# Token routing between attention and a mixture of experts: scatters ahead of gathers, weight splits moved, ranks in bf16

## The chip, the cores and the metric

The kernel runs on one core of a Trainium2 chip. The metric is the device time of one execution in microseconds (us); lower is better. The core has five engines that run their own instruction streams and meet at semaphores: TensorE (PE), VectorE (DVE), ScalarE (ACT), GpSimd (POOL) and SyncE (SP), which here only issues transfers.

## What is computed

The reference, cut to what matters:

```python
# attention, q, k, v: (4, 8, 576, 64)
scores = scale * q @ k.T
scores = where(scores >= max(scores) - tau, scores, -1e9)
x = (softmax(scores) @ v)                    # -> (2304, 512)
# mixture of experts: w1 (8, 512, 1024), w2 (8, 1024, 512)
logits = x @ w_gate                          # (2304, 8)
expert_idx = argmax(logits, axis=1)
gate_w = softmax(logits)[expert_idx]
for e in range(8):
    xe = x[expert_idx == e]
    out[expert_idx == e] = gate_w * (maximum(xe @ w1[e], 0) @ w2[e])
# second network: w_in (512, 2048), w_out (2048, 512)
h = out @ w_in
result = (h - tanh(h)) @ w_out
```

Each token goes to exactly one expert, and which one is known only after attention.

## The kernel before

**Stages.** Attention runs over 16 pairs of heads (`PAIRS`), each in 9 units of score rows. Then comes the routing, then the experts in 25 tiles of 128 token rows (`ITEMS` = 18 + 7: the rows of an expert start at a multiple of 128), then the second network in 9 groups of 256 rows. All matrix products that matter are made in three passes of a high and a low part of each operand; so every weight chunk (128 x 2048, `CHUNK`, four for each expert) has to be split into both parts in the `ring`: a copy that rounds (high, L557) and a subtraction (low, L559), both on GpSimd for the experts.

**Attention's end.** VectorE's `scale_rows` writes the attention rows to `x_sb` and, for each head, its part of the gate logits to `lg_parts`; each counts up `x_ready`. SP's `keep_batch` copies `x_sb` to the DRAM tensor `x_tokens`, the last batch after the last `x_ready`. ScalarE issues the zero fill of `x_sorted` (`clear_rows`, L1391) near the end of attention.

**Routing, a chain on VectorE (L1176 to L1263).** The helper `step` makes each instruction wait for the one before. In order: the late logits (L1176, the last six token tiles over all eight heads), maximum, shift, `onehot` (one-hot expert for each token), `run_in` (a running count along the 18 tiles in each partition), `run_ex` (L1205). TensorE then makes three fp32 products (L942 to L944): the rank of each token among those of its expert, and the count of each expert. From the counts VectorE works out how many tiles each expert takes (`ntile`, `tile_end`), the first slot of each (`base`), the slot of each token (`slot_of`, `pos`, `pos_u` at L1226, which releases `pos_ready`). After that it finds which tokens stand in the first three tiles (`PICKED` = 3): `item_of`, `lane_of`, `in_item`, `row_at` (L1229 to L1238), and `lanes` (L1241, two instructions of nine token tiles each). TensorE multiplies `lanes` with `row_at` (L950, 18 bf16 products), VectorE turns the result into row numbers, `item_rows` (L1252 to L1255). Beside them stand the map from tile to expert (`tile_end_i` L1245, `item_e_i` L1249) and the first output row of each tile (`row0_i`, L1263).

**GpSimd's queue in this stretch (L708 to L741).** When attention is over it issues the loads of chunks 4 and 5 into `raw_mid`, splits both (`split_mid`), waits for `map_ready` and `rows_ready`, gathers the rows of the first three tiles straight from `x_tokens` (L721, indirect DMA), and only then scatters all 18 token tiles to their slots in `x_sorted` (L730, indirect DMA). After that it splits the other chunks as SP loads them (L734 on); SP starts these loads when all scatters have landed, since they land in `x_sb` (`raw_late`).

**The experts.** TensorE turns the rows of a tile (`turn_rows`, L963), ScalarE and VectorE make the high and low part (`high_xT` L1522, `low_xT` with the helper at L1267), TensorE multiplies (`up`, L974), ScalarE applies the maximum (`relu`, L1527), TensorE turns again (`turn_hidden`, L984), both parts are made again (`high_hT` L1532, `low_hT`), TensorE multiplies (`down`, L996). The first three tiles are written out, the others loop. `up` of expert e waits for the first half of its chunks in `w_ready`, `down` for all. Tiles from the fourth on are loaded from `x_sorted` by ScalarE (`load_rows`, L1518).

## Time and profile before

| | us |
|---|---|
| median of 3 runs | 1127.73 (1126.7 to 1131.57) |
| the profiled execution | 1136.3 |
| its span, first to last instruction | 1134.6 |
| TensorE busy | 1048.8 (92%) |
| VectorE busy | 680.0 (60%) |
| ScalarE busy | 454.2 (40%) |
| GpSimd busy | 779.9 (69%) |

The profile is of one execution, and all times below are in us from the start of its span. Busy time of TensorE is modelled at the ends of its instructions. A page by 40 slices shows TensorE at 90% or more in nearly all slices but those from 340 to 400 us, the routing stretch. A line of a timeline is: start, duration (us), engine, source line, operation, output and input tiles, shapes, number of instructions, and in brackets the idle time of the engine before it with what ended it.

### The profile page before, as it was taken

How to read it: one execution, taken by the hardware profiler on the slowest of the kernel's cores; microseconds unless marked ns; L12 is line 12 of the kernel's file. 1: busy time of each engine (PE TensorE's matmuls, PEld its weight loads, DVE VectorE, ACT ScalarE, POOL GpSimd, SP SyncE). 2: the span in 40 equal slices, each digit the busy share in tenths (PEclk: the TensorE clock that was granted, in tenths of full speed). 3: DMA queues.
4: the chain of work that ended last, by engine and by line, in shares of the span. 5: the costliest groups of instructions: out<-in, count | busy, mean ns of one | idle time of the engine just before them, and what ended most of it. 6: DMA issues, size and time to landing. Idle time of an engine off the chain costs nothing.

```text
span 1134.6 us, 19577 instructions
## 1 busy us (share of the span) xinstructions
PE 1048.8 (92%) x6428; PEld 874.4 (77%) x6429; DVE 680.0 (60%) x1240; ACT 454.2 (40%) x865; POOL 779.9 (69%) x731
## 2 busy tenths in 40 slices
PE   3999999999983389999999999989999999999997
PEld 2677767777762368888888888879989999999995
DVE  2777777777765413232224223877877877778774
ACT  2777777777751011221221223333333333333332
POOL 6788888766622763888699731667777776777774
PEclk9999999999997689999999999999999999999999
DMA  4444464533473362545466451000010010100000
GB/s 95 119 120 125 105 178 99 135 96 84 126 255 116 112 251 95 188 145 191 139 235 191 139 176 57 10 19 20 19 37 19 19 37 0 37 19 19 18 10 28
DMA packets 98295, 110.13 MB, mean 97 GB/s; under 512 B 62464, under 2 KB 62464, under 8 KB 97728
## 3 DMA queue, kind: packets, MB, share of 16 engines
q1 hardware_dynamic: 84320, 77.64, 23.9%
q10 hardware_dynamic: 10256, 19.46, 4.9%
q0 software_dynamic: 3664, 12.34, 2.9%
q8 instruction: 28, 0.46, 0.2%
q14 instruction: 27, 0.22, 0.1%
HBM read 67.42 MB, written 27.32 MB: 84 GB/s over the span
## 4 chain that ended last, share of the span: by engine, by line
PE 76%; DVE 7%; POOL 7%; issue 6%; ACT 2%; DMA 1%; SPq 0%; POOLq 0%; ACTq 0%; DVEq 0%
PE ps L1018 17%; PE ps L1035 15%; PE ps L996 12%; PE ps L974 11%; PE ps L845 5%; PE ps L810 5%; PE ps L824 5%; PE ps L984 2%; POOL k_low L603 2%; POOL q_dup L590 1%; PE ps L831 1%; PE ps L857 1%; POOL thresh L610 1%; PE ps L963 1%; DVE lanes L1241 1%
## 5 line engine op out<-in xcount | busy, mean ns | idle before, releaser
L1018 PEld LDWEIGHTS ps<-x2T,ring 128*128 128x128 f32 x1728 | 217.2, 193 | 12.4 <-DVE x2T L1267 7.6
L1018 PE MATMUL ps<-x2T,ring 128*128 128x256 f32 x1728 | 220.1, 284 | 5.6 <-DVE x2T L1267 5.6
L1035 PE MATMUL ps<-ring,gT 128*128 128x512 f32 x864 | 210.3, 392 | 1.6 <-DVE gT L1267 1.6
L1035 PEld LDWEIGHTS ps<-ring,gT 128*128 128x128 f32 x864 | 157.6, 188 | 32.6 <-issue 1.8
L996 PE MATMUL ps<-ring,hT 128*128 x600 | 146.1, 399 | 4.3 <-DVE hT L1267 3.8
L756 POOL TENSOR_SCALAR x_sb<-h_sq 128x512 f32<-128x512 f32 x72 | 144.3, 2005 | 6.1
L974 PE MATMUL ps<-ring,xT 128*128 x600 | 144.6, 397 | 3.4 <-DVE xT L1267 3.4
L753 POOL TENSOR_SCALAR poly<-h_sq 128x512 f32<-128x512 f32 x72 | 48.4, 672 | 133.7 <-ACT h_sq L1560 123.6
L559 POOL TENSOR_TENSOR ring<-x_sb,ring 128x2048 fp32r<-128x2048 f32 x30 | 138.5, 4616 | 2.5
L1102 DVE SCALAR_TENSOR_TENSOR probs<-ps,thresh,probs 128x576 f32<-128x576 f32 x144 | 115.6, 813 | 38.6 <-ACT probs L1420 25.7
L996 PEld LDWEIGHTS ps<-ring,hT 128*128 128x128 f32 x600 | 112.6, 191 | 28.2 <-issue 5.5
L810 PE MATMUL ps<-k_hl,q_dup 128*128 128x288 f32 (+1 forms) x640 | 118.7, 316 | 15.7 <-DMA k_hl<-k_low 12.1
L974 PEld LDWEIGHTS ps<-ring,xT 128*128 128x128 f32 x600 | 112.3, 191 | 26.2 <-issue 4.0
L1094 DVE TENSOR_REDUCE neg_max<-ps 128x1 f32<-128x576 f32 x144 | 106.7, 750 | 30.6 <-PE ps L810 30.2
L1420 ACT ACTIVATE probs<-ps,neg_max 128x576 f32<-128x576 f32 x144 | 104.8, 740 | 17.0 <-DVE neg_max L1094 16.1
L810 PEld LDWEIGHTS ps<-k_hl,q_dup 128*128 128x128 f32 (+1 forms) x640 | 93.2, 192 | 17.1 <-issue 15.9
L755 POOL TENSOR_TENSOR poly<-poly,h_sq 128x512 f32<-128x512 f32 x72 | 98.2, 1364 | 6.0
L1568 ACT ACTIVATE gT<-poly 128x512 fp32r<-128x512 f32 x72 | 45.6, 634 | 140.1 <-PE ps L1035 94.7
L1560 ACT ACTIVATE h_sq<-ps 128x512 f32<-128x512 f32 x72 | 43.0, 597 | 138.1 <-PE ps L1018 138.1
L557 POOL TENSOR_SCALAR ring<-x_sb 128x2048 fp32r<-128x2048 f32 x30 | 57.2, 1907 | 58.1 <-SPq L525 30.0
L824 PE MATMUL ps<-ident,probs 128*128 128x128 f32 x576 | 90.6, 280 | 6.4 <-ACT pT_b L1446 4.1
L1532 ACT ACTIVATE hT<-ps 128x512 fp32r<-128x512 f32 x50 | 27.3, 596 | 164.3 <-DVE y_sb L1291 134.9
(162 smaller groups left out, 1492.6 us busy)
## 6 DMA issues: line engine op xcount, KB each, us to landing
x_sb<-in_moe_w_dram SPq DMA_DIRECT2D x26, 1024.0 KB, 5.9
q_dup<-q_dup SPq DMA_DIRECT2D x32, 288.0 KB, 3.7
x_sorted<-y_sb ACTq DMA_DIRECT2D x1, 6425.0 KB, 21.5
y_ranked<-y_sb ACTq DMA_DIRECT2D x25, 256.5 KB, 3.6
xs<-x_sorted ACTq DMA_DIRECT2D x22, 257.0 KB, 2.8
k_hl<-k_low SPq DMA_DIRECT2D x32, 160.0 KB, 2.4
xs<-y_ranked SPq DMA_DIRECT2D x8, 513.0 KB, 3.7
q_in<-in_q_dram SPq DMA_DIRECT2D x32, 128.0 KB, 2.7
```

Source lines behind the costliest of these rows:

```text
L559: pool.tensor_tensor(ring[:, low:low + CHUNK], raw, ring[:, high:high + CHUNK].bitcast(F32), ALU.subtract).then_inc(w_ready, 1)
L755: pool.tensor_tensor(poly[:, b, :], poly[:, b, :], h_sq[:, b, :], ALU.mult).then_inc(poly_ready, 1)
L756: pool.tensor_scalar(is_large[:, b, :], h_sq[:, b, :], T_SQ, None, ALU.is_ge).then_inc(large_ready, 1)
L810: mm = pe.matmul(scores_of(n)[0:rows, c, :], q_dup[:, s, a, f, cols], k_hl[:, s, a, k0 + c * CH:k0 + (c + 1) * CH], start=(f == 0), stop=( ...
L824: mm = pe.transpose(turn_bank[:, j * P:(j + 1) * P], probs_of(n)[:, k0 + j * P:k0 + (j + 1) * P], ident[:, :])
L974: mm = pe.matmul(psS[:, 0, n, :], xT[:, px, c * P:(c + 1) * P], ring[:, bass.ds(lo + (pw * SLOT + c * F + n * 512), 512)], start=(c == 0 a ...
L996: mm = pe.matmul(psO[:, 0, :], hT[:, px, c * P:(c + 1) * P], ring[:, bass.ds(lo + (pw * SLOT + DC * F + c * DM), DM)], start=(c == 0 and p ...
L1018: mm = pe.matmul(hid(b)[:, fc * GW:(fc + 1) * GW], ring[:, at:at + P], x2T[:, px, c, :], start=(c == 0 and px + pw == 0), stop=(c == DC - ...
L1035: mm = pe.matmul(out_bank(j), gT[:, b % 2, px, cols], ring[:, at:at + DM], start=(b == 0 and fc == 0 and px + pw == 0), stop=(b == NB - 1 ...
L1094: dve.tensor_reduce(neg_max[:, n % 4:n % 4 + 1], scores_of(n), AX.XY, ALU.max, negate=True).then_inc(nmax_ready, 1)
L1102: dve.scalar_tensor_tensor(out=by_halves(probs_of(n)), in0=scores_of(n), scalar=thresh[:, b:b + 1], in1=by_halves(probs_of(n)), op0=ALU.is ...
L1420: act.activation(by_halves(probs_of(n)), scores_of(n), ACT.Exp, bias=neg_max[:, n % 4:n % 4 + 1]).then_inc(exp_ready, 1)
```

## The change

Eight edits. Scatters: the first four of the 18 are issued when `pos_ready` is up, then come the three gathers, then the other 14. Chunks 4 and 5 are loaded by SP during the last pair of attention (with the tensors in the ring laid out anew to make room), their high halves are made by ScalarE (`high_mid`), and GpSimd makes the low halves behind the scatters. The late logits are reduced over six heads before the last `scale_rows`, and the last two heads are added afterwards. `run_ex` falls away: `before` becomes a matrix of 0 and -1, so that the inclusive count serves. The count product is the first of three, all in bf16, with a release of its own. Tile counts are rounded by adding and subtracting a large constant instead of by integers. Small tensors of the last steps lie in PSUM (`route_bank`). The picked rows are summed in one column by 36 products instead of 18, and VectorE copies them out in one step. TensorE waits for `row0_ready` before the first tile, ScalarE no longer waits for `w_ready`.

```diff
@@ sync
                     keep_batch(p // HP - 1)
+            last = PAIRS - 1
+            sp.wait_ge(scores_ready, UNITS * last)
+            sp.wait_ge(raw_trans, 3 * PAIRS)
+            sp.wait_ge(q_split, 2 * PAIRS)
+            sp.wait_ge(k_split, 2 * PAIRS)
+            for a in range(2):
+                sp.wait_ge(k_spread[last % 2][a], 16 * (last // 2 + 1))
+            for j in range(CHUNKS, EARLY):
+                sp.dma_start(chunk_like(raw_mid[:, j % 2, :], ...), ...).then_inc(mid_landed[j % 2], 16)
             keep_batch(B - 1)
@@ gpsimd
             def split_mid(j):
-                pool.wait_ge(mid_landed[j % 2], 16 * ((j - CHUNKS) // 2 + 1))
-                split(*divmod(j, CHUNKS), raw_mid[:, j % 2, :])
+                pool.wait_ge(w_high, j + 1)
+                pool.tensor_tensor(ring[:, low:low + CHUNK], raw_mid[:, j % 2, :],
+                                   ring[:, high:high + CHUNK].bitcast(F32), ALU.subtract).then_inc(w_ready, 1)
...
-            for j in range(CHUNKS, EARLY):
-                if j == CHUNKS:
-                    pool.wait_ge(x_ready, 2 * PAIRS)
-                pool.dma_start(chunk_like(raw_mid[:, j % 2, :], ...), ...).then_inc(mid_landed[j % 2], 16)
-            for j in range(CHUNKS, EARLY):
-                split_mid(j)
+            pool.wait_ge(s_zero_filled, 16)
+            pool.wait_ge(token_numbers, 5)
+            pool.wait_ge(x_ready, 2 * PAIRS)
+            pool.wait_ge(pos_ready, 1)
+            for t in range(BEFORE_PICKED):
+                sort_tile(t)
             pool.wait_ge(x_kept, 32 * B)
-            pool.wait_ge(map_ready, 2)
             pool.wait_ge(rows_ready, 1)
             for t in range(PICKED):
                 pool.indirect_dma_start(...)
...
-            for t in range(TILES):
-                pool.indirect_dma_start(out=x_sorted[:, :], ...).then_inc(x_scattered, 16)
+            for t in range(BEFORE_PICKED, TILES):
+                sort_tile(t)
+            for j in range(CHUNKS, EARLY):
+                split_mid(j)
@@ tensor
-            pe.matmul(psO[:, 1, 0:E * TILES], before[:, :], onehot[:, :, :], start=True, stop=False)
-            pe.matmul(psO[:, 1, 0:E * TILES], ones[:, :], run_ex[:, :, :], start=False, stop=True)
-            pe.matmul(psT[:, 0, 0:E], ones[:, :], run_in[:, :, TILES - 1], start=True, stop=True
+            pe.matmul(psT[:, 0, 0:E], ones_b[:, :], run_in[:, :, TILES - 1], start=True, stop=True
+                      ).then_inc(ranks_ready, 1)
+            pe.matmul(psO[:, 1, 0:E * TILES], not_before[:, :], onehot[:, :, :], start=True, stop=False)
+            pe.matmul(psO[:, 1, 0:E * TILES], ones_b[:, :], run_in[:, :, :], start=False, stop=True
                       ).then_inc(ranks_ready, 1)
             for t in range(TILES):
                 pe.wait_ge(lanes_ready, t // HT + 1)
-                mm = pe.matmul(psS[:, 1, 0, 0:2 * PICKED], lanes[:, t, :], row_at[:, t, :, :]...)
+                for x in range(2):
+                    mm = pe.matmul(psS[:, 1, 0, 0:PICKED], lanes[:, t, :], row_at[:, t, x, :], ...)
...
             pe.wait_ge(map_ready, 2)
+            pe.wait_ge(row0_ready, 1)
             turn_rows(0, first_rows[0])
@@ vector
+            late_heads = route_bank[:, 320:...]
+            half_item, item_of, lane_of = (route_bank[:, x * 32:x * 32 + TILES] for x in range(3))
+            in_item = route_bank[:, 128:...]
...
                     gate_logits(0, FULL - JT).then_inc(logits_ready, 1)
+                    dve.wait_ge(x_ready, 2 * (PAIRS - 1))
+                    dve.tensor_reduce(logits[:, FULL - JT:, :], lg_parts[:, FULL - JT:, 0:H - 2, :]..., AX.X, ALU.add)
                 if past:
                     scale_rows(p - 1, 1)
...
-            gate_logits(FULL - JT, TILES).then_inc(logits_ready, 1)
+            step(dve.tensor_tensor(late_heads, lg_parts[:, FULL - JT:, H - 2, :], lg_parts[:, FULL - JT:, H - 1, :], ALU.add))
+            step(dve.tensor_tensor(logits[:, FULL - JT:, :], logits[:, FULL - JT:, :], late_heads, ALU.add))
...
-            dve.tensor_tensor(run_ex[:, :, :], run_in[:, :, :], onehot[:, :, :], ALU.subtract).then_inc(runs_ready, 1)
+            dve.sem_inc(runs_ready, 1)
...
-            step(dve.tensor_scalar(count_i[:, :], psT[:, 0, 0:E], float(P - 1), float(P), ALU.add, ALU.max))
-            step(dve.tensor_scalar(ntile_i[:, :], count_i[:, :], P.bit_length() - 1, None, ALU.arith_shift_right))
-            step(dve.tensor_copy(ntile[:, :], ntile_i[:, :]))
+            step(dve.tensor_scalar(counts[:, 0, :], psT[:, 0, 0:E], 1.0, (P - 1) / 2, ALU.max, ALU.add))
+            step(dve.tensor_scalar(counts[:, 1, :], counts[:, 0, :], 1 / P, WHOLE, ALU.mult, ALU.add))
+            step(dve.tensor_scalar(ntile[:, :], counts[:, 1, :], WHOLE, None, ALU.subtract))
...
-            step(dve.tensor_scalar(item_of_i[:, :], pos_u[:, :].bitcast(I32), P.bit_length() - 1, None, ALU.arith_shift_right))
-            step(dve.tensor_copy(item_of[:, :], item_of_i[:, :]))
+            step(dve.tensor_scalar(half_item, pos[:, :], (P - 1) / 2, 1 / P, ALU.subtract, ALU.mult))
+            step(dve.tensor_scalar(item_of, half_item, WHOLE, WHOLE, ALU.add, ALU.subtract))
...
             dve.tensor_copy(tile_end_i[:, :], tile_end[:, :]).then_inc(map_ready, 1)
+            dve.wait_ge(rows_psum, 1)
+            dve.tensor_copy(item_rows[:, :], psS[:, 1, 0, 0:PICKED]).then_inc(rows_ready, 1)
+            # then item_ge, item_e, item_e_i, wasted, item_ge, lost, row0, row0_i
@@ scalar
+            act.wait_ge(x_ready, 2 * PAIRS)
+            act.wait_ge(w_high, CHUNKS)
+            high_mid(CHUNKS)
             act.wait_ge(lshift_ready, 1)
             act.activation(lexp[:, :, :], logits[:, :, :], ACT.Exp).then_inc(lexp_ready, 1)
+            for j in range(CHUNKS + 1, EARLY):
+                high_mid(j)
...
             act.wait_ge(map_ready, 2)
-            act.wait_ge(w_ready, EARLY)
             act.wait_ge(row0_ready, 1)
```

`high_mid(j)` waits for `mid_landed` and copies `raw_mid[:, j % 2, :]` to the high part of the ring, then counts up `w_high`; `sort_tile(t)` is the scatter of one token tile, as it was.

## Rows read from the trace of the kernel before

**Rows 1.** The page's first line.
```profile
span 1134.6 us, 19577 instructions
```

**Rows 2.** Windows by stage: stretch, us, busy of each engine, TensorE clock, DMA share, GB/s.
```profile
357.00:365.00 8.00, 1.52 (x6) 1.46 (x6) 6.29 (x22) 0.00 (x0) 1.89 (x1) 0.50 0.85 302
...
460.00:712.00 252.00, 252.00 (x1262) 211.76 (x1260) 76.36 (x126) 60.96 (x106) 176.68 (x59) 1.00 0.48 161
```

**Rows 3.** Timeline of VectorE, 340 to 430 us.
```profile
352.80 0.42 DVE L1117 TENSOR_TENSOR x_sb<-ps,rec 128x256 f32<-128x256 f32 x1 [8.53 <-PE ps L857]
...
353.75 0.84 DVE L1133 TENSOR_REDUCE logits<-lg_parts 128x48 f32<-128x384 f32 x1
...
357.18 0.31 DVE L1205 TENSOR_TENSOR run_ex<-run_in,onehot 128x144 f32<-128x144 f32 x1
...
359.27 0.17 DVE L1214 TENSOR_SCALAR count_i<-ps 128x8 int32<-128x8 f32 x1 [1.05 <-PE ps L944]
...
361.81 0.18 DVE L1226 CAST pos_u<-pos 128x18 uint32<-128x18 f32 x1
...
362.65 0.22 DVE L1234 TENSOR_TENSOR in_item<-item_of,item_no 128x54 f32<-128x54 f32 x1
...
363.16 1.86 DVE L1238 TENSOR_SCALAR row_at<-in_item,partition_no 128x54 bf16<-128x54 f32 x1
365.06 8.66 DVE L1241 TENSOR_TENSOR lanes<-lane_of,lane_no 128x1152 bf16<-128x1152 f32 x2
373.64 4.46 DVE L1245 CAST tile_end_i<-tile_end 128x8 int32<-128x8 f32 x1
...
379.23 0.17 DVE L1255 CAST item_rows<-picked_rows 128x3 uint32<-128x3 f32 x1
...
380.27 0.21 DVE L1263 CAST row_i<-row 128x25 int32<-128x25 f32 x1
...
396.29 0.69 DVE L1267 TENSOR_TENSOR xT<-ps,xT 128x512 fp32r<-128x512 f32 x1 [9.97 <-issue]
```

**Rows 4.** Timeline of GpSimd, 320 to 480 us.
```profile
363.08 1.89 POOL L557 TENSOR_SCALAR ring<-raw_mid 128x2048 fp32r<-128x2048 f32 x1 [7.30 <-DMA raw_mid<-in_moe_w_dram]
365.05 4.49 POOL L559 TENSOR_TENSOR ring<-raw_mid,ring 128x2048 fp32r<-128x2048 f32 x1
369.52 3.00 POOL L557 TENSOR_SCALAR ring<-raw_mid 128x2048 fp32r<-128x2048 f32 x1
372.60 5.47 POOL L559 TENSOR_TENSOR ring<-raw_mid,ring 128x2048 fp32r<-128x2048 f32 x1
380.26 1.10 POOL L721 DMA_INDIRECT xs<-x_tokens,item_rows  x1 [2.19 <-DVE item_rows L1255]
...
406.01 0.97 POOL L730 DMA_INDIRECT x_sorted<-x_sb,pos_u  x1 [0.30 <-issue]
```

**Rows 5.** Timeline of TensorE, 345 to 430 us.
```profile
373.78 0.40 PE L950 MATMUL ps<-row_at,lanes 128*128 128x6 bf16 x9 [2.56 <-DVE lanes L1241]
383.79 1.08 PE L963 MATMUL ps<-ident,xs 128*128 128x128 f32 x4 [9.61 <-DMA xs<-x_tokens,item_rows]
...
407.20 1.45 PE L996 MATMUL ps<-ring,hT 128*128 x4 [3.78 <-DVE hT L1267]
409.03 7.67 PE L996 MATMUL ps<-ring,hT 128*128 x20 [0.38 <-issue]
...
423.26 5.71 PE L996 MATMUL ps<-ring,hT 128*128 x24
```

**Rows 6.** Timeline of ScalarE, second half of the first hidden tile.
```profile
405.56 0.60 ACT L1532 ACTIVATE hT<-ps 128x512 fp32r<-128x512 f32 x1 [5.06 <-remote]
```

**Rows 7.** Timeline of GpSimd, first split of expert 2's chunks.
```profile
447.67 1.91 POOL L557 TENSOR_SCALAR ring<-x_sb 128x2048 fp32r<-128x2048 f32 x1 [19.24 <-SPq L525]
```

**Rows 8.** DMA issues, 310 to 345 us and the page: line, engine, count, size, us to landing.
```profile
x_sorted<-y_sb ACTq DMA_DIRECT2D x1, 6425.0 KB, 21.5
x_tokens<-x_sb SPq DMA_DIRECT2D x4, 1024.0 KB, 4.9
```

More of the change, by code:

```diff
@@ L54, in attention_moe_mlp @@
     PICKED = 3
+    BEFORE_PICKED = 4
     LAG = 3
@@ L128, in attention_moe_mlp @@
         zeros = y_sb
-        (before, ones, logits, lmax, lexp, lsum, rev, pick, pick_max, onehot, keep, item_no, item_ge, item_e,
-         run_in, run_ex, count_i, ntile_i, ntile, tile_end, base, slot_of, pos, lane_no, tile_no, partition_no,
-         picked_rows, item_of_i, item_of) = at_once([
+        (before, not_before, ones_b, logits, lmax, lexp, lsum, rev, pick, pick_max, onehot, keep, run_in, slot_of,
+         item_no, item_ge, item_e, counts, ntile, tile_end, base, ones, pos, lane_no, tile_row, partition_no) = at_once([
             ("before", [P, P], F32),
-            ("ones", [P, P], F32),
+            ("not_before", [P, P], BF16),
+            ("ones_b", [P, P], BF16),
             ("logits", [P, TILES, E], F32),
@@ L146, in attention_moe_mlp @@
             ("item_e", [P, ITEMS], F32),
-            ("run_in", [P, E, TILES], F32),
-            ("run_ex", [P, E, TILES], F32),
-            ("count_i", [P, E], I32),
-            ("ntile_i", [P, E], I32),
+            ("counts", [P, 2, E], F32),
             ("ntile", [P, E], F32),
@@ L949, in _ @@
                 pe.wait_ge(lanes_ready, t // HT + 1)
-                mm = pe.matmul(psS[:, 1, 0, 0:2 * PICKED], lanes[:, t, :],
-                               row_at[:, t, :, :].rearrange("p x i -> p (x i)"),
-                               start=(t == 0), stop=(t == TILES - 1))
+                for x in range(2):
+                    mm = pe.matmul(psS[:, 1, 0, 0:PICKED], lanes[:, t, :], row_at[:, t, x, :],
+                                   start=(t == 0 and x == 0), stop=(t == TILES - 1 and x == 1))
             mm.then_inc(rows_psum, 1)
```

133 lines of the change are left out of this document (70 added, 63 removed).

## Prediction

> **What bounds the kernel now.** I first read the page of the profile for the shares, then the windows by stage, then the chain of waits in order of time, and last the timelines of the single engines around the place where TensorE is idle. The span is 1134.6 us [rows 1]. In the expert stage TensorE has no idle time at all: busy 252.00 of 252 us at full clock [rows 2]. So nothing that the change does to ScalarE, VectorE or GpSimd there can show, unless it makes TensorE wait. The place that counts is the routing between attention and the first expert tile. From 357 to 365 us TensorE is busy for 1.52 of 8 us at a granted clock of 0.50, its 1.2 GHz level [rows 2]. The chain runs through VectorE from 353.75 (the late logits) to 379.40 (`item_rows`, 379.23 + 0.17), then through the first gather of GpSimd at 380.26, and TensorE turns its rows at 383.79 [rows 3 to 5]. What follows is bound by TensorE, so a shift of that 383.79 should reach the end of the kernel whole.
>
> In that chain the eye falls on three VectorE steps. A copy of 54 elements per partition takes 1.86 us, two of 1152 take 8.66 together, one of 8 elements takes 4.46 [rows 3], while their neighbour L1234 of 54 elements takes 0.22. GpSimd is splitting weights from 363.08 on, and the ends fit to 0.1 us: L1238 ends at 365.02, GpSimd's first split instruction at 364.97; the last split ends at 378.07, `tile_end_i` at 378.10 [rows 3, 4]. The second `lanes` step releases TensorE at 373.78 [rows 5], 1.26 after the third split instruction ended (372.52), so a `lanes` step alone costs about 1.2. The engines take turns for whole instructions. The Trainium skill (SBUF — State Buffer, "Who interferes with whom") says the same of a VectorE step with two SBUF inputs, or of a copy or cast between SBUF tensors; by that rule, the trace agrees.
>
> **The change, part by part.** All times are on the axis of the profiled execution.
>
> (a) Late logits. The reduction of 384 elements (0.84 at 353.75) becomes two additions of 48 elements on the path, priced by L1234 (54 elements, 0.22, and 0.02 to the next): 0.48 in place of 0.87, so -0.39. The six other heads are reduced before the last `scale_rows`, in an idle stretch of 8.53 us before 352.80 [rows 3]: at most 0.84, hidden ten times over.
>
> (b) `run_ex` goes: -0.32 (357.18 to 357.50). VectorE then idles 1.05 before L1214 for the three fp32 products [rows 3]. Now one bf16 product of 8 columns must land within the three softmax steps (some 0.8 us). Nine bf16 products of such a size take 0.40 [rows 5]; I take the idle time as gone. At worst it stays: 0 to -1.05.
>
> (c) Five steps of 8 elements in place of seven. From 359.27 to 360.69, the start of L1222, seven take 1.42, so two less give -0.41. The magic-number rounding costs the same per step. Positions are now ready at 361.99 (361.81 + 0.18) [rows 3]; (a) to (c) give -2.17: 359.82.
>
> (d) GpSimd's queue. Today it is: two chunk loads, two splits, three gathers, 18 scatters. After the change: four scatters, three gathers, 14 scatters, two half splits. The indirect DMAs start every 1.29 us ((406.01 - 380.26) / 20), and the first came 0.86 after its release (379.40 to 380.26) [rows 3, 4]. So: first scatter 359.82 + 0.86 = 360.68; four take 5.15: 365.83; the first gather starts then; its rows reach TensorE 3.53 later (380.26 to 383.79): **369.4 in place of 383.8**. The gather now lies behind four scatters in its queue: between nothing and one period, 1.29. I take nothing, since a scatter is issued only every 1.29 us. The gathers' other condition, the kept copy, is issued at x_ready and takes 4.9 [rows 8]; done near 359.5.
>
> (e) Whether the picked rows are known by then. From 359.82: three steps of 18 elements (0.21 each, by L1226), three of 54 (0.25): 361.2. Two `lanes` steps of 1.2: 363.6. Products for the second half are 18 now, not 9: 0.80 and 0.1 of hand-over: 364.5. One copy out of PSUM in place of three steps: 364.8 [rows 3, 5]. That is 1.0 us ahead of the gather, so the four scatters and not VectorE set the gather's start; the longer list of products costs 0.4, which this 1.0 covers.
>
> (f) TensorE now also waits for `row0_ready`, with eight map steps after `item_rows`. Today's steps of that kind take 0.2 to 0.36; eight come to 2.3: 367.1, against 369.4. Hidden by 2.3 us; nothing is queued behind this wait on TensorE but the first item.
>
> (g) Chunk loads on SP during the last pair. They come after the loads of v; in the queue behind them is only the last kept copy, due at 353.7. The zero fill of 6.4 MB needs 21.5 us at that time [rows 8]; 2 MB more lengthens it by about a third, 7 us, so to some 344, still 16 before the first scatter. No cost. The added constant on GpSimd at the start, two short steps, is not on the chain I read; I take 0, at most 0.3.
>
> (h) ScalarE makes the high halves. One of 2048 elements per partition is at most four times 0.60 (512 elements, [rows 6]) = 2.4, from 353.75 to 356.2; then `lexp`, 0.3, used near 356.9. Hidden by 0.4; the bound of the miss is 0.5. GpSimd's two low halves, 4.5 each [rows 4], now start after the scatters, at 365.83 + 17 x 1.29 = 387.7, and end near 397. Expert 1 uses them only after the tiles of expert 0: today GpSimd waits until 447.67 for SP's release of expert 0's first half (SPq L525) [rows 7]. 50 us of margin.
>
> **Sum.** 369.4 - 383.8 = -14.4 us (a shift of the start, not the sum of the single steps). With the bounds of (b), (d) and (h): -14.4 to -11.6; below, -15.2, if the 0.86 before the first indirect DMA is mostly the wake-up of a queue whose other conditions now come first. The profiled execution took 1136.3 us, so 1121.9. It is 8.6 above the median of the runs shown, 1127.73; I keep that distance: **1113.3**.
>
> **The rivals.**
>
> *Late releases shrink* (faster still). In [rows 6] ScalarE's copy of the second half of the first hidden tile starts at 405.56 after 5.06 us that no engine's record explains. TensorE then idles 3.78 before 407.20, and the 24 products run to 416.70, 9.5 in place of 5.71 with a warm clock [rows 5]. That is 7.6 us, beside the scatters, which end at 407 [rows 4]. Now 14 and not 18 scatters lie beside the first items. If the stall goes whole: 1105.7. Against: TensorE's first items and the remaining scatters start together as before; and the profiled run is 8.6 over the median, so the stall may not be in the timed runs.
>
> *Descriptors take turns with VectorE* (less gain). Splits and VectorE's steps within SBUF exclude each other in [rows 3, 4]; the indirect DMAs may do so too. Five map steps have only SBUF operands (`item_ge` twice, `item_e_i`, `row0`, `row0_i`), each exposed to a descriptor step of 0.97: row0 is ready at 367.1 + 4.9 = 372.0, TensorE starts 2.6 later: 1115.9. Against it: L1263 took 0.21 at 380.27, right beside the gather that ran from 380.26 to 381.36 [rows 3, 4]. The Trainium skill (SBUF — State Buffer, "SBUF: two separate sides") states this rule for software DMAs beside copies within SBUF; it speaks against putting scatters beside the map steps, and that one row does not bear it out.
>
> *Late releases reach the start* (much less gain). The 5.06 of [rows 6] could strike the event of the last picking product, since four scatters now run beside it, and once more that of the first turned tile. Rows would be known at 369.9, TensorE would start 3.53 later, 373.5, and lose 5.06 again: 9.2 of the 14.4 are gone: 1122.5. Against: today TensorE's first tile, up to 396.29, meets no such wait beside the first 12 scatters [rows 3].
>
> *Every VectorE step waits for a descriptor step* (slower). If steps with one SBUF operand are caught too, ten steps to `item_rows` take 12.9: 372.7; the gathers then stand behind four scatters and rows land at 377; eight map steps end at 383.0. So the 14 us are gone; and seven VectorE steps of items 0 and 1, up to 0.97 each beside 14 scatters, add 6.8: 1127.7 - 0.7 + 6.8 = 1133.8. It decides from 0.97 per step in about 20 of the 25 steps. Against: the step at 396.29, one operand in PSUM, took its ordinary 0.69 in the middle of the scatters [rows 3, 4].
>
> **How the numbers follow.** Forecast 57% (1112.5 to 1116.1), stall gone 20% (1105.7), map steps held 12% (1115.9), late start 8% (1122.5), slower 3% (1133.8). The range takes in the first three, with 1 and 3 us for the distance between profiled and timed: 1105 to 1119. About 0.5% (5.6 us) is what a measurement can tell from no change; below 1122.1 lie the first three and a quarter of the fourth: 91%; within 7%; slower by more 2%.
>
> **What would show it.** Right: `pos_u` ends near 359.8, the two `lanes` steps take 1.2 each, no VectorE step of 8 elements takes over 0.3, first scatter at 360.7, TensorE's first L963 at 369.4, the expert stage without idle time. Wrong: `item_rows` later than the fourth scatter's end; `row0_i` after the gather's landing; any new idle time of TensorE at expert 1's first tile; a stall at the hidden tile of another length than before.

## The result, and where its time lies

The kernel before takes 1129.78 us (median of five runs, 1126.7 to 1131.57), the changed kernel 1119.27 us (median of five, 1118.12 to 1121.1): the ratio is 0.9912, with an interval of 0.9891 to 0.9933. That is 10.5 us less. The forecast was 14.4 us less, 1113.3 us; the measured time lies 0.3 us above the upper end of its range. Of the 6.0 us between 1113.3 and 1119.27, 2.05 are the base (the forecast started from 1127.73, the median of three runs, and five give 1129.78); the other 3.9 are gain that did not come.

The profiled execution of the changed kernel took 1119.28 us. The first line of its page:

```profile
span 1117.5 us, 19613 instructions
```

Against [rows 1] the span is 17.1 us shorter, more than the 10.5 of the timed medians. Two places make it up. TensorE's first tile is turned at 373.55 and not at 383.79 [rows 5], which is 10.24 earlier. From there to the end of the first item's second matrix (the product with `hT`) it takes 25.2 us and not 32.9. That second difference of 7.7 is the stall of [rows 6], which the profiled execution of before has and that of after does not. After it both need nearly the same, 717.9 and 718.8 us. So 10.24 is the change's own part, and it agrees with the timed 10.5. The profiled execution of before (1136.3) lay 6.5 us above the median of its five timed runs, and the stall is of that size; that the timed runs mostly went without it is inferred from this and not shown.

VectorE's timeline of the changed kernel, from the last attention output to the end of the map (start, us, line, operation, operands; in brackets the idle time before it and what ended it):

```profile
354.58 0.22 DVE L1209 TENSOR_TENSOR ps<-lg_parts 128x48 f32<-128x48 f32 x1
...
356.70 0.78 DVE L1222 TENSOR_TENSOR onehot<-pick,pick_max 128x144 bf16<-128x144 f32 x1
357.52 0.46 DVE L1226 TENSOR_TENSOR_SCAN run_in<-keep,onehot 128x144 bf16<-128x144 f32 x1
358.12 0.30 DVE L1231 TENSOR_REDUCE lsum<-lexp 128x18 f32<-128x144 f32 x1
...
358.96 0.17 DVE L1237 TENSOR_SCALAR counts<-ps 128x8 f32<-128x8 f32 x1
...
361.09 0.18 DVE L1248 CAST pos_u<-pos 128x18 uint32<-128x18 f32 x1
...
362.34 0.28 DVE L1259 TENSOR_SCALAR row_at<-ps,partition_no 128x54 bf16<-128x54 f32 x1
362.65 2.62 DVE L1262 TENSOR_TENSOR lanes<-ps,lane_no 128x1152 bf16<-128x1152 f32 x2
...
365.19 0.16 DVE L1265 CAST tile_end_i<-tile_end 128x8 int32<-128x8 f32 x1
366.01 0.16 DVE L1268 CAST item_rows<-ps 128x3 uint32<-128x3 f32 x1 [0.66 <-PE ps L965]
...
368.07 0.20 DVE L1282 CAST row_i<-row 128x25 int32<-128x25 f32 x1
```

The long steps of [rows 3] are gone: `row_at` takes 0.28 in place of 1.86, the two `lanes` steps 2.62 together in place of 8.66, and `tile_end_i` 0.16 in place of 4.46. The item rows are known at 366.17, 4.90 after the positions (361.27); before it was 17.4 (361.99 to 379.40).

GpSimd and TensorE of the same execution:

```profile
364.50 1.23 POOL L726 DMA_INDIRECT x_sorted<-x_sb,pos_u  x1 [20.72 <-issue]
366.03 0.98 POOL L726 DMA_INDIRECT x_sorted<-x_sb,pos_u  x1 [0.30 <-issue]
...
369.86 0.99 POOL L739 DMA_INDIRECT xs<-x_tokens,item_rows  x1 [0.30 <-issue]
...
373.55 1.09 PE L977 MATMUL ps<-ident,xs 128*128 128x128 f32 x4 [7.58 <-DMA xs<-x_tokens,item_rows]
...
393.01 5.72 PE L1010 MATMUL ps<-ring,hT 128*128 x24
```

The first scatter starts 3.23 us after the positions are ready. That is the one large surprise, and the chain of waits shows it as time in which nothing is seen to run:

```profile
361.09 0.19 DVE pos_u L1248
...
361.30 0.04 POOLq L733
361.35 3.15 issue
364.50 1.23 POOL x_sorted L726
```

GpSimd's sequencer passed its wait for the positions (L733) at 361.30, and 3.15 us later the first scatter began. From there on all goes by the forecast: the fourth scatter ends, the gather follows, its rows land, TensorE turns them.

### The profile page after: what moved, and what is told of

Read it like the earlier page. It is cut to its first block, busy times and chain, and to the rows that moved or that the text cites. A ratio compares the mean times of both kernels' runs of the same rounds, so it can differ in the third digit from the quotient of the medians.

```text
span 1117.5 us, 19613 instructions
## 1 busy us (share of the span) xinstructions
PE 1046.8 (94%) x6443; PEld 873.4 (78%) x6444; DVE 666.2 (60%) x1238; ACT 457.5 (41%) x867; POOL 771.9 (69%) x729
## 3 DMA queue, kind: packets, MB, share of 16 engines
q0 software_dynamic: 3120, 10.24, 2.5%
## 4 chain that ended last, share of the span: by engine, by line
PE 77%; POOL 9%; DVE 6%; issue 5%; ACT 2%; DMA 1%; SPq 0%; POOLq 0%; ACTq 0%; DVEq 0%
PE ps L1032 17%; PE ps L1049 16%; PE ps L988 13%; PE ps L1010 12%; PE ps L858 5%; PE ps L837 4%; PE ps L823 4%; POOL k_low L618 2%; PE ps L998 2%; POOL q_dup L605 2%; POOL thresh L625 1%; PE ps L844 1%; PE ps L870 1%; PE ps L977 1%; POOL k_hl L616 1%
## 5 line engine op out<-in xcount | busy, mean ns | idle before, releaser
L1010 PE MATMUL ps<-ring,hT 128*128 x600 | 143.0, 394 | 0.0
L1355 DVE SCALAR_TENSOR_TENSOR poly<-poly,h_sq 128x512 f32<-128x512 f32 x72 | 50.6, 703 | 71.1 <-POOL poly L768 71.1
## 6 DMA issues: line engine op xcount, KB each, us to landing
x_sorted<-y_sb ACTq DMA_DIRECT2D x1, 6425.0 KB, 26.5
```

Source lines behind the costliest of these rows:

```text
L1010: mm = pe.matmul(psO[:, 0, :], hT[:, px, c * P:(c + 1) * P], ring[:, bass.ds(lo + (pw * SLOT + DC * F + c * DM), DM)], start=(c == 0 and p ...
```

## The experiments

Three things were open: what the 3.15 us are, which part of the change brings the gain, and whether the stall of [rows 6] belongs to one order of the GpSimd queue. For the first there were three theories. **Cold queue**: the first software DMA after a long idle time of GpSimd takes three microseconds to start. **VectorE**: the item steps of VectorE, which run without a gap behind `pos_u`, keep GpSimd from making the descriptors. **Code fetch**: the code of GpSimd behind the wait isn't loaded yet when the wait ends.

### The kernel before, once more

No edit; it shows how the stall varies.

> The kernel before once more, unchanged, to see whether its stall at the first hidden tile (TensorE idle 3.8 us before down(0), its 24 products 9.5 us instead of 5.7) stands in every execution. Theory A, the stall belongs to the profiled execution only by chance: it is absent or of another length here, and the span is up to 7 us shorter than 1134.6. Theory B, it belongs to the kernel: the ScalarE copy of the second hidden half again starts some 5 us late, and the span is within 2 us of 1134.6.

One run took 1139.55 us; the kernel before, timed eleven times in this series, had a median of 1137.1 us (1133.85 to 1139.0), some 7 us above the 1129.78 of the first. The stall is there again. ScalarE's copies out of the first hidden tile, and TensorE behind them:

```profile
401.88 0.60 ACT L1532 ACTIVATE hT<-ps 128x512 fp32r<-128x512 f32 x1 [4.38 <-remote]
408.91 0.60 ACT L1532 ACTIVATE hT<-ps 128x512 fp32r<-128x512 f32 x1 [6.43 <-remote]
...
410.55 8.28 PE L996 MATMUL ps<-ring,hT 128*128 x24 [4.24 <-DVE hT L1267]
```

The copy of the second half waits for 6.43 us. The one semaphore that ScalarE waits for there, `hT_psum`, is counted up by TensorE's turning products (L984), and the last of these ended at 396.52, 12.4 us before the copy starts; no engine's record explains the time between. TensorE idles 4.24 and then runs its 24 products at 8.28 in place of 5.71. Positions came 8.27 after the last attention output, as in the first profile.

### One indirect DMA ahead of the wait for the positions

```diff
             pool.wait_ge(x_ready, 2 * PAIRS)
+            pool.wait_ge(warm, 1)
+            pool.indirect_dma_start(
+                out=warm_dst[:, :], out_offset=None, in_=w_gate[:, :],
+                in_offset=bass.IndirectOffsetOnAxis(ap=warm_rows[:, 0:1], axis=0)).then_inc(warmed, 16)
             pool.wait_ge(pos_ready, 1)
...
             pool.wait_ge(x_kept, 32 * B)
+            pool.wait_ge(warmed, 16)
             pool.wait_ge(rows_ready, 1)
```

> The changed kernel with one small gather (8 numbers per partition, its result is not used) issued by GpSimd as soon as attention is over, before it waits for the positions. In the changed kernel the first scatter starts 3.2 us after the positions are ready, not 0.86. Theory 1, a first indirect DMA costs some 2.4 us once, or GpSimd has to wake from a long idle stretch: the small gather pays it, the first scatter starts about 0.8 us after the positions, TensorE's first tile comes 2.4 us earlier, and the time falls by 2.4 us against the changed kernel. Theory 2, VectorE's steps beside it hold GpSimd up: still 3.2 us, and no change of the time.

Measured: 1118.81 us, ratio 0.9848 (0.9827 to 0.987) to the 1137.1 of its series.

```profile
358.88 1.24 POOL L739 DMA_INDIRECT warm_dst<-in_moe_w_gate_dram,warm_rows  x1 [14.18 <-issue]
362.69 1.01 POOL L731 DMA_INDIRECT x_sorted<-x_sb,pos_u  x1 [2.56 <-DVE pos_u L1258]
```

The first scatter now starts 0.29 after the positions (362.40). The 3.2 us have moved to the dummy gather: its wait for the attention output ended at 355.71, and it started 3.17 later. Both "cold queue" and "code fetch" say this, so the run excludes only "VectorE" as the sole cause. TensorE begins 16.82 after the last attention output, in the changed kernel 18.99. The changed kernel was not timed in this series, so what this is worth in time is not known.

One more row of this kernel matters below:

```profile
368.12 0.16 DVE L1278 CAST item_rows<-ps 128x3 uint32<-128x3 f32 x1 [1.64 <-PE ps L975]
```

The last picking product ended at 367.10, and VectorE's copy of its result starts 1.02 later. In the changed kernel that is 0.04 (365.97 and 366.01). So a late release struck on the way to TensorE's start here, and the gather had to wait 1.57 for the rows.

### The gathers ahead of all scatters

```diff
-    BEFORE_PICKED = 4
+    BEFORE_PICKED = 0
```

> The changed kernel with no scatter ahead of the three gathers (BEFORE_PICKED 0). Picked rows are known at 366.1 in the profile of the changed kernel, the first gather starts at 369.86. Theory 1 (a start-up of about 3.2 us for whatever indirect DMA comes first after idling): the gather starts at about 369.3, the gain is 0.5 us at most. Theory 2 (VectorE's lanes steps delay the first one): it starts 0.9 to 1.3 us after the rows, near 367.2, and TensorE begins 2.7 us earlier; the last scatter ends at most 4 us later than before, which no one waits for.

```profile
367.44 1.23 POOL L739 DMA_INDIRECT xs<-x_tokens,item_rows  x1 [23.35 <-DVE item_rows L1268]
```

GpSimd had been idle for 23.35 us, longer than in the changed kernel (20.72), and yet its first indirect DMA started 0.91 after the rows were known (366.53). "Cold queue" falls with this row: the same first use of the queue after the same idle costs 0.9. What differs is that GpSimd had passed the wait for the positions 5 us before and stood at the next one. The DMA view between 361.5 and 364 us has one packet in it, and it is an instruction packet:

```profile
GB/s 0 0 0 0 0 0 0 0 0 0 0 0 0 0 0 0 0 0 0 0 131 0 0 0 0 0 0 0 0 0 0 0 0 0 0 0 0 0 0 0
...
q14 instruction: 1, 0.01, 1.2%
```

It lies in slice 21 of 40, at 362.8, about 1.05 after GpSimd passed the wait for the positions (361.7): here the fetch and what follows it hide under the wait for the rows.

Time: 1126.04 us, 0.9907 (0.9888 to 0.9926) of 1137.1. TensorE starts 16.18 after attention, 2.8 earlier than in the changed kernel, but the stall is back (the 24 products with `hT` take 8.44 after 3.75 idle), and that raised the question whether scatters behind the gathers cause it.

### VectorE silent while the first scatter is issued

```diff
+            dve.wait_ge(first_scatter, 16)
```

The wait stands behind `pos_u` and ahead of the item steps; the first scatter has a semaphore of its own for it.

> The changed kernel with VectorE waiting, once the positions are ready, until the first scatter has landed, so that no VectorE step runs beside the start of the first scatter. Theory 2 (the steps of VectorE hold GpSimd's first descriptors up): the first scatter starts 0.9 us after the positions. Theory 1 (start-up of its own): still about 3.2 us. In both cases the rest of the routing is some 5 us later, which is the price of the wait and is not the question.

One run, 1123.04 us: positions at 360.83, and

```profile
363.93 1.23 POOL L727 DMA_INDIRECT x_sorted<-x_sb,pos_u  x1 [19.64 <-issue]
...
367.54 0.18 DVE L1253 TENSOR_SCALAR ps<-pos 128x18 f32<-128x18 f32 x1 [6.71 <-DMA x_sorted<-x_sb,pos_u]
```

With VectorE idle for 6.71 us the first scatter still comes 3.10 after the positions. "VectorE" falls. The instruction packet is there again, 1.05 after the wait. TensorE starts at 376.65, late because of the wait put in.

### The changed kernel, once more

> The changed kernel once more, unchanged, on the chip on which the next ones run, as their yardstick. The first scatter starts 3.2 us after the positions again (3.15 in its first profile, in two kernels made from it 3.07 and 3.10 before their first indirect DMA), and TensorE's first tile starts 10 us earlier than in the kernel before. Theory A, the stall at the first hidden tile comes and goes from execution to execution: the timed gain differs from that of the first measurement (10.5 us) by some us. Theory B: 10.5 us again within its interval of 2.4.

1120.41 us (1119.94 to 1120.75), ratio 0.9909 (0.9893 to 0.9926) to a before of 1130.48 in this series. The first scatter comes 3.23 after the positions, TensorE starts 19.25 after attention, and there is no stall (17.98 from the start to the second matrix of the first item, 23.72 to its end). It is the kernel that the next three are held against.

### Eight short instructions on GpSimd, far ahead

```diff
+            filler = sb("filler", [P, 8], U32)
...
+            for i in range(8):
+                pool.memset(filler[:, i:i + 1], 0)
```

They stand at the start of the kernel, some 300 us before the routing. They compute nothing that is used; they only shift all later code of GpSimd by eight instructions.

> The changed kernel with eight tiny memsets added to GpSimd's start, which do nothing but push its later instructions eight places further. In the four profiles that show it, an 8 KB instruction fetch goes over the DMA 1.06 us after GpSimd has passed one certain wait (361.30 to 362.37 in the changed kernel), and the indirect DMA behind it starts 2.1 us after that. Theory 3, the 3.2 us are the load of GpSimd's next block of code, which begins right behind the wait for the positions: with the filler the block begins earlier, the load falls into GpSimd's idle stretch, the first scatter starts 0.9 us after the positions, TensorE's first tile 2.3 us earlier, and the time is 2.3 us shorter than that of after_again. Theory 1, a start-up of the first indirect DMA: no change at all.

```profile
361.02 1.23 POOL L729 DMA_INDIRECT x_sorted<-x_sb,pos_u  x1 [17.21 <-DVE pos_u L1251]
```

Positions are ready at 360.06, the first scatter starts 0.97 after them in place of 3.23. What the DMA queues carried around the wait, first in the changed kernel from 360 to 365 us, then with the filler from 358 to 363:

```profile
GB/s 0 0 0 0 0 0 0 0 0 0 0 0 0 0 0 0 0 0 66 0 0 0 0 0 0 0 0 0 0 0 0 0 0 0 0 0 0 0 0 0
DMA packets 1, 0.01 MB, mean 2 GB/s; under 512 B 0, under 2 KB 0, under 8 KB 0
...
q14 instruction: 1, 0.01, 0.7%
```

```profile
DMA packets 21, 0.09 MB, mean 17 GB/s; under 512 B 0, under 2 KB 0, under 8 KB 21
...
q0 software_dynamic: 21, 0.09, 4.4%
```

In the changed kernel a single packet of some 8 KB of instructions moves at 362.3, 1.06 after the wait was passed, and the scatter starts 2.1 after it. With the filler there is no such packet, only the rows of the first scatter. The instruction packets of this queue (q14) between 270 and 440 us begin at 322.2, 339.6 and 362.35 in the changed kernel, and at 315.4, 322.6 and 339.8 with the filler: one has gone from behind the wait, and one has come under attention, where nothing waits for it. (The kernel with three scatters ahead, below, has the same filler, and there they begin at 315.2, 321.6 and 339.9.) "Code fetch" stands: the same instructions at other places in the code start 2.26 us sooner. Time: 1116.87 us (1113.95 to 1117.26), ratio 0.987 (0.9848 to 0.9893), 3.5 us less than the changed kernel in the same series. At TensorE's start 1.55 of the 2.26 is seen in the profile (17.70 after attention in place of 19.25), since the gathered rows reached TensorE 4.64 after the gather's start here. The last attention output also came 2.3 earlier, which the filler can't be credited with. So the 2.26 is shown by the row, and what the timed 3.5 has above it is not accounted for.

### The splits alone moved

The kernel before, with its two splits of the middle chunks behind the 18 scatters and nothing else of the change:

```diff
-            for j in range(CHUNKS, EARLY):
-                split_mid(j)
...
             for t in range(TILES):
                 ...
+            for j in range(CHUNKS, EARLY):
+                split_mid(j)
```

(`raw_mid` moves beside them to storage that stays free until then, and ScalarE no longer waits for the splits ahead of the items.)

> The kernel before with one part of the change alone: GpSimd's two splits stand behind the scatters, and ScalarE no longer waits for them (raw_mid lies elsewhere, since it is read later). If the shared turns of GpSimd and VectorE are the bulk of the old chain, the lanes steps take 1.3 each, tile_end_i 0.2, the picked rows are known near 367.6 in place of 379.4, and TensorE starts 11 to 12 us earlier than in the kernel before, more than the 10.2 of the whole change, since no scatters stand ahead of the gathers. If the splits were not the cause, the steps keep their 1.9, 4.3 and 4.5 us.

```profile
365.58 2.63 DVE L1239 TENSOR_TENSOR lanes<-lane_of,lane_no 128x1152 bf16<-128x1152 f32 x2
368.12 0.16 DVE L1243 CAST tile_end_i<-tile_end 128x8 int32<-128x8 f32 x1
...
369.41 0.17 DVE L1253 CAST item_rows<-picked_rows 128x3 uint32<-128x3 f32 x1
```

1119.4 us, ratio 0.9909 (0.9885 to 0.9932): the whole gain of the change, in this series 1120.41 against 1119.4. The start falls from 30.07 (or 29.90) to 18.17 after attention. The `lanes` steps have all operands in SBUF here and take 2.63, just as with the operand in PSUM. So the operand in PSUM, the bf16 ranks, the steps saved and the four scatters ahead, taken together, bring nothing on top: positions come at 6.72 and not 8.26 after attention in the changed kernel, but the 3.23 before the first scatter and the four scatters ahead of the gather use up those 1.5 us and 1.1 more (19.25 and 18.17).

### The one-hot matrix in fp32

```diff
+        not_before = sb("not_before_wide", [P, P], F32)
+        onehot = sb("onehot_wide", [P, E, TILES], F32)
...
-        (before, not_before, ones_b, logits, lmax, lexp, lsum, rev, pick, pick_max, onehot, keep, run_in, slot_of,
+        (before, _, ones_b, logits, lmax, lexp, lsum, rev, pick, pick_max, _, keep, run_in, slot_of,
```

> The changed kernel with onehot in fp32 instead of bf16 (and the matrix of 0 and -1 with it). The step that writes onehot took 0.40 us in the kernel before and 0.78 in the changed one. If the write of 2-byte elements 36 bytes apart is the cause, it takes 0.40 again and the positions are ready 0.3 us earlier after the end of attention, or less where the fp32 product takes longer. If the layout of the tensors is the cause, it stays at 0.78.

```profile
356.39 0.41 DVE L1224 TENSOR_TENSOR onehot_wide<-pick,pick_max 128x144 f32<-128x144 f32 x1
```

One run, 1117.85 us: the step takes 0.41 in place of 0.78, and positions come 6.34 in place of 6.72 after attention, 0.38 less. The product in fp32 hides as well as the one in bf16. The time of a single run proves nothing about 0.38 us; the row shows it.

### The three together, with three scatters ahead

```diff
-    BEFORE_PICKED = 4
+    BEFORE_PICKED = 3
```

with the filler and the fp32 matrix of the two kernels above.

> The changed kernel with the filler of eight memsets, onehot in fp32, and three scatters ahead of the gathers instead of four. Filler: the scatters start 0.97 after the positions. Three of them end their issue 5.0 us after the positions, and the picked rows are known 4.9 after them, so the first gather is bound by the rows: it starts 5.75 us after the positions, 0.6 earlier than with four. From the start of the last logits step to TensorE's first tile: before 30.0 us, changed kernel 19.0, with the filler 17.7; expected here 16.7. Time: 3 to 4 us below the changed kernel, ratio to the kernel before about 0.986. If the filler's gain was noise: ratio 0.990.

```profile
366.94 0.98 POOL L744 DMA_INDIRECT xs<-x_tokens,item_rows  x1 [0.94 <-DVE item_rows L1273]
...
370.32 1.08 PE L982 MATMUL ps<-ident,xs 128*128 128x128 f32 x4 [4.39 <-DMA xs<-x_tokens,item_rows]
```

1113.46 us (1111.1 to 1115.31), ratio 0.9847 (0.9831 to 0.9863): the fastest of all kernels here. TensorE starts 15.45 after attention. The gather now waits 0.94 for the item rows: with three scatters ahead VectorE sets the start, with four the scatters would (the gather 0.65 later, 362.21 + 1.53 + 3 x 1.28 = 367.6). The start accounts for 3.8 of the 7 us to the changed kernel (19.25 and 15.45); in the profiles 0.7 more lie ahead of the end of attention and 2.6 behind TensorE's start, and no run says what the latter are (from the end of the first item's second matrix on, these profiles differ by as much: 717.5 us here, 720.1 in the changed kernel's).

### The gathers first, in another series

> The changed kernel with no scatter ahead of the gathers, once more. In its first profile TensorE's first tile came 2.8 us earlier than in the changed kernel, but it stalled 3.75 us at the first hidden tile, at the lower clock afterwards, as the kernel before did in that session (1137.1 us); the later session, with the kernel before at 1130.5, showed no such stall in four kernels. Theory S, the stall belongs to the session and not to the order of the DMAs: where the kernel before is near 1130 here, this kernel shows no stall and runs at a ratio of 0.988. Theory O, it belongs to the 18 scatters that now lie beside the first tiles: the stall is there again and the ratio is 0.991 whatever the session.

1116.62 us, ratio 0.9876 (0.9861 to 0.9891), where the same kernel took 1126.04 before. The start is the same, 16.24 and 16.18. The stall is not there:

```profile
390.36 5.72 PE L1010 MATMUL ps<-ring,hT 128*128 x24
```

Held against the kernel before of its own series, this order is 14.0 us faster (1130.64 and 1116.62), the changed kernel 10.1 (1130.48 and 1120.41), and the splits alone moved 11.1. So the four scatters ahead of the gathers cost, 3.0 us at TensorE's start (19.25 and 16.24), while the other parts of the change together bring about 3 us on top of the splits. Part of the 3.0 is the code fetch, which shows only when a scatter stands directly behind the wait for the positions: with the filler and four scatters the start was 17.70, 1.5 later than here.

The stall, then, does not belong to an order of the queue. In every profile of the two series in which before took 1130.5 and 1130.6 it is absent; in the series with before at 1137.1 it costs both gathers-first and before, and two others (the dummy gather, VectorE silent) show a late release of 4.4 us, with TensorE idle about 1 us. It is not the series alone either: the first profile of before has the stall, and the runs timed beside it had a median of 1129.78.

### The operands in PSUM alone

The kernel before with `lane_of` and `in_item` in PSUM, the splits left where they are:

```diff
-        lane_of = sb("lane_of", [P, TILES])
+        lane_of = route_bank[:, 0:TILES]
+        item_in_psum = route_bank[:, 128:128 + TILES * PICKED].rearrange("p (t x) -> p t x", x=PICKED)
```

> The kernel before with one part of the change alone: lane_of and in_item lie in PSUM, the splits stay beside VectorE's chain. If only a VectorE step with two SBUF inputs, or a copy or one-input step within SBUF, takes turns with GpSimd, then the row_at step of 1.86 us takes 0.3 and the two lanes steps 1.3 each in the middle of the splits, while tile_end_i, SBUF to SBUF, still waits until a split ends. The map steps behind it wait in their turn, so the picked rows come only some 3 us earlier (near 376.6), and so does the first tile, since ScalarE still waits for the second split (376): gain 1 to 3 us. If PSUM operands do not help, nothing changes.

```profile
363.71 1.88 DVE L1236 TENSOR_TENSOR ps<-item_of,item_no 128x54 f32<-128x54 f32 x1
...
365.89 0.28 DVE L1240 TENSOR_SCALAR row_at<-ps,partition_no 128x54 bf16<-128x54 f32 x1
366.21 2.62 DVE L1243 TENSOR_TENSOR lanes<-ps,lane_no 128x1152 bf16<-128x1152 f32 x2
368.74 1.40 DVE L1247 CAST tile_end_i<-tile_end 128x8 int32<-128x8 f32 x1
...
370.42 0.34 DVE L1250 TENSOR_REDUCE item_e<-item_ge 128x25 f32<-128x175 f32 x1
370.79 1.38 DVE L1251 CAST item_e_i<-item_e 128x25 int32<-128x25 f32 x1
...
372.27 4.47 DVE L1255 SCALAR_TENSOR_TENSOR picked_rows<-picked_rows 128x3 f32<-128x3 f32 x1
```

```profile
365.61 4.51 POOL L561 TENSOR_TENSOR ring<-raw_mid,ring 128x2048 fp32r<-128x2048 f32 x1
370.08 2.06 POOL L559 TENSOR_SCALAR ring<-raw_mid 128x2048 fp32r<-128x2048 f32 x1
372.23 4.49 POOL L561 TENSOR_TENSOR ring<-raw_mid,ring 128x2048 fp32r<-128x2048 f32 x1
```

The operand in PSUM does what it is for: both `lanes` steps run at 2.62 in the middle of a split of 4.51, where [rows 3] has 8.66. But steps whose inputs are in SBUF now wait in their place: `tile_end_i` 1.40, `item_e_i` 1.38, and a step of 3 elements takes 4.47, as long as the split beside it. `in_item` (L1236) waits too, 1.88, though its result goes to PSUM: both its inputs are in SBUF. Not every step within SBUF waits: the reduction `item_e` took its usual 0.34 inside a split instruction (370.08 to 372.14). 1128.36 us, ratio 0.9982 (0.9972 to 0.9991): 2.3 us, against 11 for moving the splits. The Trainium skill (SBUF — State Buffer, "Who interferes with whom") puts the line between VectorE steps that use the ports shared with GpSimd (two SBUF inputs, or copies and casts within SBUF in certain modes) and those that do with VectorE's own, among them reductions; by that rule, the trace agrees, in these rows.

## Why the prediction was wrong in its number and right in its course

The difference to the forecast is 4.19 us at TensorE's start (373.55, and 369.36, which the prediction rounds to 369.4). The measured start lies 1.3 us outside the prediction's own bounds for it (-14.4 to -11.6, and it was -10.24). The difference has five terms.

**The first scatter, step (d): +2.37.** This is the step that failed. It took 0.86 from [rows 4] as the time from a release to the first indirect DMA and set it behind the positions. In the kernel before that 0.86 was measured at the gather, when the code was long in place: the last instruction packet ahead of it begins at 358.7, while GpSimd stood at the wait for chunk 4 (355.8 to 363.1), and the gather came at 380.26. Here the packet moved only when the wait for the positions had been passed, and the first scatter took 3.23. The runs show it from three sides: it stays with VectorE silent (3.10), it is gone after a longer idle time behind another wait (0.91), and it is gone when the code is shifted by eight instructions (0.97). The prediction saw that the 0.86 might change here, but only downwards (its -15.2, if the 0.86 was mostly a wake-up); upwards it had one period of 1.29 for the gather behind the scatters, and nothing for the first scatter itself.

**The end of attention: +0.83.** The last output was complete at 354.56 and not at 353.73. The last 20 products of attention took 5.40 in place of 4.46, because TensorE's granted clock was at its 1.2 GHz level for 6.8 and not for 3.4 us there. The same varies between executions of kernels that differ nowhere near it: the repeated kernel before, the one with VectorE silent and the one with the filler run these products in 4.30 to 4.61 us, the changed kernel twice (5.40 and 5.60) and the one with only the splits moved (5.60) in the longer time. The last of these has the chunk loads where before has them, so step (g), chunk loads during attention at no cost, is not contradicted. The zero fill landed after 26.5 us in place of 21.5, at about 342; (g) had said 344.

**The positions, steps (a) to (c): +0.62.** (a) gave 0.38 (353.75 to 354.62 before, 354.58 to 355.07 now), as forecast. (c) gave 0.41 (2.72 and 2.31 us from the first count to the end of `pos_u`), as forecast. (b) took `run_ex` and the idle time at 1.37 and got 1.14; TensorE is done in time, and `lsum` starts 0.14 after `run_in`. Not foreseen at all was the price of writing `onehot` as bf16: 0.78 in place of 0.40 us. The prediction had no term for the narrower type, and the experiment gave the 0.38 back.

**Four scatters, +0.21, and the gather, +0.16.** The first scatter's period was 1.53, not 1.29, and the rows reached TensorE 3.69 after the gather's start, not 3.53.

**What held.** (e): item rows 4.90 after the positions, forecast 5.0; `lanes` at 1.3 each, forecast 1.2. The four scatters and not VectorE set the gather's start, as forecast; the rows were known 3.7 before it, where the forecast had 1.0. (f): the map done 7.0 after the positions, forecast 7.3, hidden. (h): the two high halves lie on ScalarE beside the routing, the exponentials are used 1.4 after they are made, and the low halves on GpSimd run late and without anyone waiting:

```profile
354.58 1.91 ACT L1534 ACTIVATE ring<-raw_mid 128x2048 fp32r<-128x2048 f32 x1 [2.05 <-DVE lg_parts L1143]
356.40 0.31 ACT L1540 ACTIVATE lexp<-logits 128x144 f32<-128x144 f32 x1
...
391.32 9.17 POOL L578 TENSOR_TENSOR ring<-raw_mid,ring 128x2048 fp32r<-128x2048 f32 x2
```

The shift of the start reaches the end of the kernel whole, as forecast: 10.24 at the start, 10.5 in the medians.

**The rivals.** *Descriptors take turns with VectorE* did not happen. The eight map steps, all but `wasted` with all operands in SBUF, ran from 366.08 to 368.27 beside the second and third scatter at 0.15 to 0.34 us each, and `tile_end_i` beside the first at 0.16. (One step elsewhere may have been held for 0.2 us: in the fp32 kernel `tile_end_i` took 0.36 and ended with the first scatter.) *Every VectorE step waits for a descriptor step* falls with it, and the experiment with VectorE silent shows that the other direction isn't there either. *Late releases reach the start*: `item_rows` starts 0.66 after VectorE's step before it and 0.04 after the picking product's end, so the release came in time. The rival is not empty, though: in the kernel with the dummy gather this release came 1.02 after the product's end, in one of the nine profiles that have this step. It cost about 1 us there and not the 5.06 that the prediction gave it. *Late releases shrink*: the stall is indeed absent from the profiled execution of after (5.72 for the 24 products, no idle time before them), but 10.5 us in the medians beside 10.24 at the start leave no room for it in most timed runs of before, so it gave the ratio next to nothing; it comes and goes between series and executions and not with the kernel. What makes the release late remains open: ScalarE's second copy starts 9.2 to 12.4 us after the last turning product's end in the three profiles where TensorE stalls, and nothing shows why. Gathers-first took 9.4 us more in the series at 1137.1 than in the one without the stall (1126.04 and 1116.62); its kernel before took 6.5 more.

The measured 1119.27 thus belongs to none of the five cases that the prediction priced; it lies between its 1115.9 and its 1122.5. That it came within 0.3 us of the range is owed to the 3 us that the range gives to the distance between profiled and timed runs, not to a term for what happened; from the base of 1127.73 the same gain would have landed at 1117.2, inside it.

## What to carry to other kernels

Where a chain of short VectorE steps has splits or copies of GpSimd beside it, moving those out of the chain is the gain (11.9 of 30 us here, by the one edit); giving some of the steps an operand in PSUM hands most of the wait to the next steps within SBUF (2.3 us). Work that nobody waits for yet belongs ahead of the transfer that everybody waits for only as far as it fits under what that transfer waits for anyway: four scatters and the fetch in front of them made the start 3.0 us later, three scatters without the fetch were over before the rows were known. Before a release is priced by the time that another release took on the same engine, look at where the engine's code is fetched: an instruction packet in the DMA view just behind a long wait, with an unexplained gap up to the next instruction, was 2.3 us here, and eight instructions far ahead moved the fetch under earlier work. And an operation counted as free because its type gets smaller has to be looked up in a row of that very form.

## What the runs showed of the hardware that was not expected

- In the changed kernel GpSimd did not fetch its next block of code (one packet of some 8 KB) while it stood idle for 17.5 us, the last 6.7 of them at the wait for the positions; the packet moved 1.0 to 1.1 us after the wait in front of it was passed in all seven profiles that have it there, and where nothing else hid it the next instruction came 3.1 to 3.2 after the release in place of 0.97. Standing at a wait does not stop a fetch as such: in gathers-first, and in the kernel before at 358.7, the packet moved during a wait. The Trainium skill (Runtime: NRT & Kernel Launch, "Instruction fetch mechanics") describes blocks of 16 KiB that are fetched while the current one runs, so that crossing a border is mostly hidden. Here GpSimd's packet is half that size and the crossing behind a wait is not hidden; the measurement decides.
- VectorE's write of 144 bf16 elements per partition into `onehot` took 0.78 us, of 144 fp32 elements 0.40 to 0.41, from the same fp32 operands. The scan that wrote `run_in`, in order, took 0.46 in both types, so it is not the type alone; `onehot` is written transposed, with 18 elements between neighbours, and fp32 written so is fast, so it is not the spacing alone either. The same step writing bf16 in order was not tried.
- The instructions that issue indirect DMAs (0.97 to 1.23 us each on GpSimd) did not hold VectorE's steps within SBUF for their length (0.15 to 0.34 us each in the changed kernel; the most seen anywhere is 0.2 us of delay), though a split instruction on the same engine holds such steps for its whole length (4.47 beside 4.49).
- The same kernel's level moved by 7 us between two series on the same chip (1137.1 and 1130.5). The profiles of the slower series show late releases at the first hidden tile, those of the faster one none; that these make up the 7 us is not shown.
